# When the split w_out blocks are kept for reloading, and when batches 2 and 3 of the pooled attention are turned: two tables of one fused kernel

## The reference

```python
def sm_attn(qq, kk, vv):                     # softmax(scale * qq kk^T) vv
    ...
# q, k, v: (4, 8, 576, 64); factor = 4
q_d, k_d, v_d = (t.reshape(B, H, 144, 4, D).mean(axis=3) for t in (q, k, v))
out_up = np.repeat(sm_attn(q_d, k_d, v_d), 4, axis=2)          # pooled attention
mask = np.abs(pos[:, None] - pos[None, :]) < 4                 # local attention
out_local = softmax(np.where(mask, scale * q @ k.T, -1e9)) @ v
x = (out_up + out_local).transpose(0, 2, 1, 3).reshape(2304, 512)
y = ((x @ w_a) * (x @ w_b)) @ w_out          # 512 -> 1536 -> 512
h = y @ w_in                                 # 512 -> 1024
solu = h * softmax(h)
out = ((solu - mean) / np.sqrt(var + 1e-6) * g_ln) @ w_out2    # 1024 -> 512
```

## Time and profile before

| | |
|---|---|
| median of 3 runs | 805.56 us (803.61 to 807.89) |
| the profiled execution | 805.56 us, of which the span from first to last instruction is 803.8 us |
| PE busy | 774.4 us, 96% of the span |
| DVE, ACT, POOL busy | 70%, 38%, 27% |
| the chain that ended last, by engine | PE 90%, DVE 3%, POOL 2%, DMA, ACT and issue 1% each |
| granted TensorE clock, mean | 0.992 |

### The profile page before, as it was taken

The page is one execution under the profiler, slowest core; times in us unless marked ns, Lnnn a source line. Parts: engine busy times, 40 slices in busy tenths (PEclk is TensorE's granted clock), DMA queues, the critical chain, the costliest instruction groups (busy, mean ns, idle before and its releaser), DMA issues.

```text
span 803.8 us, 12202 instructions
## 1 busy us (share of the span) xinstructions
PE 774.4 (96%) x4392; PEld 708.1 (88%) x4392; DVE 560.5 (70%) x992; ACT 304.2 (38%) x824; POOL 216.7 (27%) x261
## 2 busy tenths in 40 slices
PE   5879899899999999999999999999999999999998
PEld 4758789899899999999899999999988888888886
DVE  1479998978988787868677886112457676676663
ACT  3453545435353525244253524224422222212212
POOL 3449866718324503023001211111200000000000
PEclk9999979999999999999999999999999999999999
DMA  9999947665977685684755443456120111111111
GB/s 183 214 222 255 225 97 239 209 187 189 285 221 226 230 234 158 169 218 117 180 188 171 149 159 109 142 185 210 53 66 31 50 52 39 42 53 42 37 40 39
DMA packets 94539, 118.86 MB, mean 148 GB/s; under 512 B 17041, under 2 KB 56723, under 8 KB 94481
## 3 DMA queue, kind: packets, MB, share of 16 engines
q1 hardware_dynamic: 79760, 108.59, 47.6%
q10 hardware_dynamic: 14721, 9.51, 4.1%
HBM read 97.23 MB, written 20.84 MB: 147 GB/s over the span
## 4 chain that ended last, share of the span: by engine, by line
PE 90%; DVE 3%; POOL 2%; DMA 1%; ACT 1%; issue 1%; ACTq 1%; DVEq 0%; POOLq 0%
PE psum L842 27%; PE psum L844 26%; PE psum L843 26%; PE psum L778 2%; PE psum L956 2%; PE psum L798 2%; PE psum L690 1%; DMA wo_raw<-in_moe_w_out 1%; PE psum L809 1%; PE psum L788 1%; POOL raw L1673 1%; ACTq L997 1%; PE psum L710 1%; POOL wo_lo L1693 0%; PE psum L765 0%
## 5 line engine op out<-in xcount | busy, mean ns | idle before, releaser
L842 PE MATMUL psum<-x_hi,w_hi 128*128 128x384 f32 x576 | 200.3, 348 | 0.6 <-DVE x_lo L1362 0.4
L844 PE MATMUL psum<-x_hi,w_lo 128*128 128x384 f32 x576 | 195.1, 339 | 0.0
L843 PE MATMUL psum<-x_lo,w_hi 128*128 128x384 f32 x576 | 194.9, 338 | 0.0
L842 PEld LDWEIGHTS psum<-x_hi,w_hi 128*128 128x128 f32 x576 | 109.8, 191 | 4.4 <-issue 3.0
L843 PEld LDWEIGHTS psum<-x_lo,w_hi 128*128 128x128 f32 x576 | 110.1, 191 | 0.0
L844 PEld LDWEIGHTS psum<-x_hi,w_lo 128*128 128x128 f32 x576 | 109.8, 191 | 0.0
L1368 DVE TENSOR_TENSOR ab_f<-psum,a_sb 128x384 f32<-128x384 f32 x72 | 39.9, 555 | 95.8 <-PE psum L844 64.9
L842 PE MATMUL psum<-ab_hi,wo_hi 128*128 128x384 f32 x288 | 100.7, 350 | 0.2
L844 PE MATMUL psum<-ab_hi,wo_lo 128*128 128x384 f32 x288 | 97.3, 338 | 0.0
L843 PE MATMUL psum<-ab_lo,wo_hi 128*128 128x384 f32 x288 | 97.3, 338 | 0.0
L1673 POOL TENSOR_TENSOR raw<-raw 96x256 f32<-96x256 f32 x60 | 56.1, 960 | 127.3 <-DMA raw<-in_q 64.0
(11 more groups left out here) (144 smaller groups left out, 1452.2 us busy)
## 6 DMA issues: line engine op xcount, KB each, us to landing
wo_hi<-wo_hi_scratch SPq DMA_DIRECT2D x53, 256.0 KB, 2.8
wo_lo<-wo_lo_scratch SPq DMA_DIRECT2D x53, 256.0 KB, 3.2
k_u<-in_k SPq DMA_DIRECT2D x11, 576.0 KB
v_u<-in_v SPq DMA_DIRECT2D x11, 576.0 KB
k_u<-in_k SPq DMA_DIRECT2D x17, 288.0 KB
v_u<-in_v SPq DMA_DIRECT2D x17, 288.0 KB
wo_raw<-in_moe_w_out SPq DMA_DIRECT2D x19, 256.0 KB, 4.2
raw<-in_v SPq DMA_DIRECT2D x8, 576.0 KB, 6.7
```

The lines of the kernel that those rows point to most:

```text
L842: mm(dst, wh, xh, start=first, stop=False, skip_group_check=not check)
L843: mm(dst, wh, xl, start=False, stop=False, skip_group_check=not check)
L844: last = mm(dst, wl, xh, start=False, stop=end, skip_group_check=not check)
```

## The change

Three things are changed.

- **Which blocks are fresh and kept.** Tile 0 is fresh as before. In tile 1 the odd blocks are fresh (13, 15, 17, 19, 21, 23) and not blocks 12 to 18. Kept are the even blocks of tile 0 (0, 2, 4, 6, 8, 10) and the odd ones of tile 1. Fresh blocks are 18 and not 19; stores are 12 pairs as before.
- **When q and k are turned.** In tile 1, q of batch 2 is turned in slot 25 and not 28. In tile 3, q of batch 3 in slot 10 and not 11, k in slot 11 and not 12, and jobs 14 and 15 begin in slots 12 and 17 and not 13 and 18.
- **Two loads of tile 3** stand one slot earlier on SP: `load_xup(4, 0)` in slot 18, `load_unit_v(4, 1)` in slot 19.

```diff
-        (3, 0, "R", 2, 0), (3, 5, "R", 2, 2), (3, 13, "R", 3, 0), (3, 18, "R", 3, 2),
+        (3, 0, "R", 2, 0), (3, 5, "R", 2, 2), (3, 12, "R", 3, 0), (3, 17, "R", 3, 2),
...
-QK_AT = {0: {10: (4, 5), 11: (6, 7)}, 1: {28: (8, 9)}, 2: {0: (10, 11)}, 3: {11: (12, 13), 12: (14, 15)}}
+QK_AT = {0: {10: (4, 5), 11: (6, 7)}, 1: {25: (8, 9)}, 2: {0: (10, 11)}, 3: {10: (12, 13), 11: (14, 15)}}
...
-FIRST_KEPT = 7
...
 def wo_fresh(g):
     m, j = divmod(g, FC)
-    return m == 0 or (m == 1 and j < FIRST_KEPT)
+    return m == 0 or (m == 1 and j % 2 == 1)
 
 def wo_kept(g):
     m, j = divmod(g, FC)
-    return wo_fresh(g) and (m == 0) == (j >= FIRST_KEPT)
+    return wo_fresh(g) and m == j % 2
...
-                            if n == (18, 13, 13, 19, 13)[m]:
+                            if n == (18 if rest else 13):
                                 load_xup(m + 1, 0)
-                            if n == (19, 14, 14, 20, 14)[m]:
+                            if n == (19 if rest else 14):
                                 load_unit_v(m + 1, 1)
```

## The result

The changed kernel takes 811.46 us (median of 7 runs, 810.25 to 814.71), the kernel before, run beside it, 803.61 us (7 runs, 802.38 to 807.89). The ratio of their runs is 1.0099, with a 95% interval of 1.0072 to 1.0127: the change costs 1.0%, about 7.9 us. The forecast was 815.5 us, +9.9.

What follows compares the result with a forecast made beforehand. PE was taken to bound the kernel, busy 774 of 803.8 us. The terms 2.0 - 1.2 - 1.1 + 5.8 + 3.4 + 1.0 = +9.9 us on 805.6 gave 815.5 us, range 807.5 to 821.5.

Steps and rivals of the forecast that it cites:

- What bounds the kernel: Whole kernel: PE is busy 774 of 803.8 us; tile waits with the clock hold about 15 us, the most removable.
- Slot 25: Tile 1: POOL does block 21 before q of batch 2, so PE waits 5.8 us; bounds 3.8 to 8.7.
- wrong if POOL's q starts before 224 us: Tile 1: sign that would refute the forecast, as would a PE wait in slot 25 below 2 us.
- Clock behind slot 25: Tile 1: PE's low clock after the wait adds 3.4 us, the mean of 1.7 and 5.2; range 1.7 to 5.2.
- Start of tile 0: Stores of blocks 0 and 2 delay the loads of blocks 3 and 4: +2.0 us, range 0 to 4.
- The clock at nothing, since the low clock is there in both: Start of tile 0: no change in clock loss, 0 us, as the low clock occurs before and after.
- End of tile 0: Without block 12 POOL ends earlier and DVE runs faster before PE's wait at 159.5: -1.2 us, range -3 to 0.
- Tile 1, first half: Without block 16 DVE's scalar is faster and most of PE's wait at 202.7 goes: -1.1 us, range -1.2 to 0.
- Tile 3: PE waits 1.6 us for q in slot 10, while 0.6 us at 400.5 goes: +1.0 us, range 0 to +3.
- Relief wins: Rival: waits at 159.5 and 202.7 go and no wait comes at slot 25: 800.7 us; chance 0.06.
- Both slow: Rival: POOL and DVE block each other for both halves of q, full clock loss: 820.2 us; chance 0.15.
- Small prices: Rival: stores cost nothing, slot 25's wait is 3.8 us, the clock costs 1.7: 809.8 us; chance 0.22.

Runs made afterwards that it cites:

- the best kernel of the study: Changed kernel with POOL's q of batch 2 ahead of block 21, k of batch 1 ahead of blocks 3 and 4, tile 3 as before: 802.53 us, ratio 0.9975.
- the run with the rule alone: Kernel before with only the new rule for fresh and kept blocks of w_out; turns and jobs as before: 807.33 us, ratio 1.0037.
- q first: Changed kernel with only POOL's order changed, both halves of q of batch 2 ahead of block 21's low part in tile 1: 803.56 us, ratio 0.9999.
- the kernel before with the turn alone: Kernel before with one number changed, q of batch 2 turned in slot 25 of tile 1 and not 28: 803.19 us, ratio 0.9995.
- the run without the two stores: Changed kernel with blocks 0 and 2 kept in tile 1, not tile 0, and blocks 12 and 14 fresh again: 811.58 us, ratio 1.0095.
- the run that joins it with q first: Changed kernel with blocks 0 and 2 kept in tile 1, POOL's q ahead of block 21, tile 3's tables and loads as before: 803.66 us, ratio 0.9992.
- the last experiment: The run without the two stores, with POOL's low part of block 3 moved behind block 4's up weights: one execution, 815.3 us, kernel before 806.66.
- the run with k first: Kernel before with POOL's halves of k of batch 1 ahead of the low parts of blocks 3 and 4 in tile 0: 803.11 us, ratio 0.9992.

## Why the prediction was right

Its size, its sign and the place of the loss held. By its own steps:

**What bounds the kernel**: right. PE's busy time fell by 1.9 us and the span grew by 4.5; the added time is PE's waits. "The change can take away no more" than some 15 us was never put to the test: the best kernel of the study won 2.0 us.

**Slot 25**: right, and the case for it was the strongest in numbers. Predicted 5.8 us, measured 5.98 (2.31 + 3.67); block 21 right ahead of q; the halves of q 6.5 and 4.1 us where 5.9 and 3.9 to 4.1 were taken. The absolute times were off: block 21's load was issued at 218.6, not 222.2, and q began at 223.5. By the letter the test "wrong if POOL's q starts before 224 us" is met and the forecast should have failed. It did not, because PE had also come some 3.5 us earlier (228.0, not 231.4), with the low clock at 101 us absent in this execution. Both ends of the wait hang on PE's own progress, so the test should have been written as a distance, POOL's start of q less than 8.3 us ahead of PE, and not as a time. The reason given for a slow first and a fast second half holds too: in the run with the rule alone PE doesn't stop until 234.1, DVE goes on, and both halves are slow, 6.5 and 7.3 us. Two slips of its arithmetic are small: 225.1 + 0.63 + 2.2 is 227.9 and not 227.6, and the slow bound is 8.8 and not 8.7. What it did not see is that the rule alone is enough for a wait at slot 28 (3.02 us): that kernel needs 13.8 us for q.

**Clock behind slot 25**: predicted 3.4 us, range 1.7 to 5.2. The clock row 232 to 240 with 0.61 gives (1 - 0.61) x 8 = 3.1 us, but part of that stretch PE is idle, where the clock costs nothing; the matmuls run at 1.2 GHz from 234.8 to 238.2, and half of these 3.4 us, 1.7 us of work, is lost, the low end of the range. The same care would have lowered the second price taken from the earlier trace rows: 1.7 us by the row, 1.2 by the matmuls. Wait and clock together are 5.98 + 1.7 = 7.7 us in the trace against 9.2 forecast; by the runs they are 7.9 - (-0.1) = 8.0, the changed kernel less the one with q first. The clock is the term that was mis-sized, 3.4 for 1.7, and 1.2 of the 2.0 us by which the sum was too high lie in these two terms, 9.2 for 8.0. Another 2.0 us of the 4.0 between 815.5 and 811.5 lie in the base, 805.6 for a median of 803.6.

**Start of tile 0**: the delay came, at half its size, and its effect on the time did not. Block 3 was split at 84.81 for 82.84, 2.0 us later, and k was turned 1.8 us later, which looks like the 2.0 of the sum. But PE was 0.7 to 1.1 us late already at 56 to 60 us, before the first store was issued at 63.8, and block 2 was split at 70.73 for 69.69. From issue to landing block 3's load took 10.65 us for 9.71, and 10.64 in the run with the rule alone, so the store costs it some 0.9 us. In that run block 2 is on time, and k is turned 0.75 us late. That the 2.0 was met is luck. Two rows of the kernel after:

```profile
84.81 0.63 ACT L1110 ACTIVATE wo_hi<-wo_raw 128x512 fp32r<-128x512 f32 x1 [4.80 <-DMA wo_raw<-in_moe_w_out]
...
91.84 0.63 ACT L1110 ACTIVATE wo_hi<-wo_raw 128x512 fp32r<-128x512 f32 x1 [3.77 <-DMA wo_raw<-in_moe_w_out]
```

"The clock at nothing, since the low clock is there in both" was wrong for this pair of profiles: the wait was now split in two, 2.54 us for ACT ahead and 0.88 for POOL, and the low clock stood behind the first, for 3.5 us of matmuls and not 9.9. That is 3.2 us of work won back. How much of this is the change and how much the one execution can be judged by the kernel before with the turn alone, which has no low clock at 100 to 112 us though it waits 2.28 us for k, which ends at 99.3:

```profile
100.00:112.00 12.00, 11.17 (x64) 9.89 (x63) 11.93 (x11) 6.42 (x22) 11.26 (x11) 1.00 0.60 139
```

The profile on which the prediction rests had caught a dear clock there, and was 2 us above the later median. The mistake is to take its clock loss as the kernel's.

**End of tile 0**: predicted -1.2, and the wait for `accT` fell from 3.13 to 1.92, -1.2, by the reason given: 0.94 us for 1.47 in DVE's row.

```profile
154.78 1.08 DVE L1368 TENSOR_TENSOR ab_lo<-ab_f,ab_hi 128x384 fp32r<-128x384 f32 x1
155.78 0.94 DVE L1462 TENSOR_TENSOR accT<-acc,xup 128x768 f32<-128x768 f32 x1
```

Of the two instructions only the second was relieved; POOL ended its row at 155.4, between them. In this execution 1.09 us came back at 162.6 for DVE's `x_lo`. It is not there in the runs with the rule alone and with q first (2.06 and 2.04 us at `accT`, nothing behind), so -1.1 is the better measure. In the run without the two stores block 12 is fresh again, and the wait is back at 3.10 us (2.47 in the run that joins it with q first). The low clock behind it, 2.4 us of matmuls before, is gone in this execution and there in the one with q first (3.6 us): the scatter again.

**Tile 1, first half**: right in size (1.16 to 0.13, forecast -1.1), wrong in the reason. DVE's scalar still takes 1.01 us beside POOL; it only starts 1 us earlier against PE, at 196.87 with PE there at 198.7, where before it was 200.68 and 201.5. Nor is the size firm: in the run with the rule alone 0.76 of the 1.16 us are still there.

```profile
196.87 1.01 DVE L1308 TENSOR_SCALAR pool_bias<-pool_max 96x2 f32<-96x2 f32 x1
```

**Tile 3**: waits of 1.5 to 1.7 us in four traces with its edits (1.6 forecast), 0.67 in the run without the stores, 0.51 in the changed kernel itself, and 0.6 gone in slot 22. Alone it can't be told from nothing.

**Sum without slot 25**: 2.0 - 1.2 - 1.1 + 1.0 = +0.7 was forecast; the run with q first holds just these terms and gives -0.1 us [-1.4, +1.4]. With 0.9 for the 2.0 the sum would be -0.4.

**Rivals.** "Relief wins" was to decide at POOL's start of q, and the run with q first is that rival made real: POOL starts q at 212.6, 6.5 us ahead of the point (227.4 - 8.3 = 219.1), and the wait is gone. The relief then pays for the stores and no more. "Both slow" fails: q took 10.6 us and not 12.4, at the low price of the clock. "Small prices" had the clock right (1.7) and the wait wrong (3.8 for 5.98): its +4.2 is farther from +7.9 than the forecast's +9.9, though its 809.8 lies nearer to 811.5, since it stands on a base that is 2 us too high.

## What to carry to other kernels

An engine that takes its work in a written order hands on the latest of its inputs: an instruction whose input another engine's progress releases holds up all that stands behind it, here ten microseconds of ready work behind two instructions that take 1.4 us together. Before a consumer is moved earlier, read what stands ahead of its producer and what that waits for; the mend was three lines of order. Price the parts together as well as one by one: the early turn cost nothing alone, and took the loss from 0.3% to 1.0% beside the new rule. And before a loss of clock is taken from one trace as a term, see whether a second execution has it.

## What the runs showed of the hardware

**The low clock differs from one execution to another, and behind waits of the same length.** At 100 to 112 us the granted clock was 0.57 behind a wait of 3.02 us and 1.00 behind one of 2.28 us; in the last experiment PE ran at 1.2 GHz for 12.6 us behind a wait of 2.87 us, and in the kernel with the rule alone for 5.3 us behind 3.02 us. The eight runs of the changed kernel had a mean clock between 0.973 and 0.994 and times from 810.1 to 814.7 us. At the end of tile 0 PE was at 1.2 GHz for 3.4 us behind a wait of 3.13 us in the kernel before; in the run with k first the clock stayed at 1.00 behind a wait of 3.12 us that ended at 154.5:

```profile
154.00:160.00 6.00, 4.55 (x27) 4.22 (x27) 6.00 (x10) 1.51 (x3) 0.00 (x0) 1.00 0.28 101
```

That execution took 800.42 us, and the median of its twelve runs was under 1 us below that of the kernel before.

**DVE can stand for the length of several instructions of POOL.** The run without the two stores has the stop of 4.89 us above and one of 4.40. DVE's timeline there:

```profile
89.47 4.40 DVE L1422 TENSOR_SCALAR u_den<-u_sum 128x12 f32<-128x12 f32 x1
```

and POOL's:

```profile
90.33 2.81 POOL L1681 TENSOR_TENSOR w_lo<-w_raw,w_hi 128x256 fp32r<-128x256 f32 x4
93.10 1.44 POOL L1689 TENSOR_TENSOR wo_lo<-wo_raw,wo_hi 128x256 fp32r<-128x256 f32 x2
```

Twelve elements a lane take 4.40 us, and POOL's four instructions in that time take 0.70 us each, as little as anywhere in these traces. In the kernel before, the same happens to two of DVE's products with v, which take 4.54 and 4.92 us for the usual 0.95 to 1.49. The first:

```profile
88.57 4.54 DVE L1443 TENSOR_TENSOR tmp<-v_u,p_u 128x768 f32<-128x768 f32 x1
```

The Trainium skill, page SBUF — State Buffer, section "SBUF: two separate sides", says that whoever starts first has the shared ports for its whole instruction and the other waits. The traces agree that DVE stops while POOL goes on at its shortest times, but the stop lasts for a row of POOL's instructions, not for one. By that section of the Trainium skill a DVE instruction takes part if it has two SBUF inputs or runs in a two-port mode; the one with twelve elements has a single input, and no trace shows its mode. At other places the two engines take turns (3.92 us for POOL's four, DVE at 0.94 to 1.48 an instruction). What chooses between turns and a long stop was not found.
